# Clustered attention before two expert layers: one-hot tiles turned three at a time, mask rows on 96 partitions, six transfers for two

## What is computed

```python
# attention: B=2, H=8, S=768, D=64, 16 clusters
q_assign = argmax(q_n @ c_n.T)          # cluster of each query, per head
k_assign = argmax(k_n @ c_n.T)          # cluster of each key
mask = q_assign[:, :, :, None] == k_assign[:, :, None, :]
scores = where(mask, scale * q @ k.T, -1e9)
attn = softmax(scores);  out = attn @ v
# experts: N=1536, D=512, E=8, F=1024
idx = argmax(xn @ en.T / tau);  out = gate * (relu(x @ w1[e]) @ w2[e])
# last: d_ff=1536
out = ((x @ w_a) * (x @ w_b)) @ w_out
```

## Time and profile before

| | us |
|---|---|
| median of 3 runs | 868.93 |
| lowest to highest | 867.5 to 874.71 |
| the profiled execution | 872.69 |
| its span, which the profile's times count from | 870.6 |
| PE busy (share of the span) | 823.5 (95%) |
| DVE busy | 424.3 (49%) |
| ACT busy | 288.9 (33%) |
| GpSimd busy | 131.7 (15%) |

### The profile page before, as it was taken

The page is one execution under the profiler, slowest core; times in us unless marked ns, Lnnn a source line. Parts: engine busy times, 40 slices in busy tenths (PEclk is TensorE's granted clock), DMA queues, the critical chain, the costliest instruction groups (busy, mean ns, idle before and its releaser), DMA issues.

```text
span 870.6 us, 13204 instructions
## 1 busy us (share of the span) xinstructions
PE 823.5 (95%) x5441; PEld 748.6 (86%) x5441; DVE 424.3 (49%) x690; ACT 288.9 (33%) x496; POOL 131.7 (15%) x125
## 2 busy tenths in 40 slices
PE   5799999999999999849999999999999999999996
PEld 4589998999989989749999999978888888888885
DVE  5746676776656763258555555544313111131111
ACT  3123323333323343445555555533213111121111
POOL 6001121211111210023333331000001000010001
PEclk9999999999979999859999999999999999999998
DMA  5212222222241101286767677640001000010001
GB/s 135 55 41 60 60 54 70 61 52 60 59 162 41 34 5 56 78 260 188 221 210 216 216 217 216 196 140 7 0 1 49 1 0 1 1 49 0 1 1 48
DMA packets 57471, 72.36 MB, mean 83 GB/s; under 512 B 17696, under 2 KB 40064, under 8 KB 57280
## 3 DMA queue, kind: packets, MB, share of 16 engines
q1 hardware_dynamic: 54624, 63.89, 24.9%
q0 software_dynamic: 2784, 7.58, 2.9%
HBM read 57.24 MB, written 6.30 MB: 73 GB/s over the span
## 4 chain that ended last, share of the span: by engine, by line
PE 90%; DVE 5%; DMA 2%; issue 2%; POOL 1%; ACT 0%; SPq 0%; POOLq 0%; ACTq 0%; DVEq 0%
PE bank L1287 14%; PE bank L1492 8%; PE bank L1494 8%; PE bank L1493 7%; PE pair L1245 5%; PE pair L1451 3%; PE pair L1453 3%; PE pair L1452 3%; PE first_pair L1271 3%; PE bank L1222 3%; PE first_pair L1273 3%; PE bank L1218 2%; PE first_pair L1512 2%; PE first_pair L1510 2%; PE first_pair L1511 2%; PE bank L1512 2%
## 5 line engine op out<-in xcount | busy, mean ns | idle before, releaser
L1287 PE MATMUL bank<-v_sb,prob 128*128 128x66 f32 x1152 | 145.7, 278 | 0.0
L1287 PEld LDWEIGHTS bank<-v_sb,prob 128*128 128x128 f32 x1152 | 144.6, 198 | 0.1
L891 DVE TENSOR_REDUCE neg_max<-pair 128x1 f32<-128x768 f32 x93 | 88.7, 954 | 73.6 <-PE pair L1245 73.5
L1177 DVE TENSOR_TENSOR g_sb<-bank,a_sb 128x512 f32<-128x512 f32 x36 | 24.9, 692 | 187.3 <-PE bank L1494 187.3
L1492 PE MATMUL bank<-x_hi,wt 128*128 128x512 f32 x288 | 112.1, 389 | 1.6 <-DVE x_lo L1158 1.6
L1494 PE MATMUL bank<-x_hi,wt 128*128 128x512 f32 x288 | 112.0, 389 | 0.0
L1493 PE MATMUL bank<-x_lo,wt 128*128 128x512 f32 x288 | 112.0, 389 | 0.0
L651 ACT ACTIVATE prob<-first_pair 128x384 f32<-128x384 f32 x128 | 59.6, 489 | 137.2 <-PE first_pair L1273 136.3
L958 DVE TENSOR_TENSOR wt<-w_raw,wt 128x2048 fp32r<-128x2048 f32 x41 | 93.6, 2287 | 15.7 <-ACT wt L686 15.7
L686 ACT ACTIVATE wt<-w_raw 128x2048 fp32r<-128x2048 f32 x41 | 78.3, 1909 | 1.7 <-DMA w_raw<-in_moe_w_dram 1.1
L1451 PE MATMUL pair<-ht_hi,wt 128*128 128x240 f32 x256 | 71.3, 279 | 0.0
(11 more groups left out here) (229 smaller groups left out, 1625.1 us busy)
## 6 DMA issues: line engine op xcount, KB each, us to landing
w_raw<-in_moe_w_dram SPq DMA_DIRECT2D x32, 1024.0 KB, 9.0
q_raw<-in_q_dram SPq DMA_DIRECT2D x16, 192.0 KB, 2.4
k_raw<-in_k_dram SPq DMA_DIRECT2D x16, 192.0 KB, 2.5
v_sb<-in_v_dram SPq DMA_DIRECT2D x16, 192.0 KB, 3.0
qb<-qa SPq DMA_DIRECT2D x16, 192.0 KB, 2.6
kc<-kd SPq DMA_DIRECT2D x16, 192.0 KB, 2.6
w_raw<-in_moe_w_a_dram SPq DMA_DIRECT2D x3, 1024.0 KB, 7.1
w_raw<-in_moe_w_b_dram SPq DMA_DIRECT2D x3, 1024.0 KB, 8.7
```

Source lines behind the costliest of these rows:

```text
L891: dve.tensor_reduce(neg_max[n % 2][:, t:t + 1], masked_in(n, t)[:, :, 0:HALF], AX.XY, ALU.max, negate=True).then_inc(mx_done, 1)
L1287: last = pe.matmul(o_tiles[:, t, :], prob[s][:, j, t * P:(t + 1) * P], v_in_sb[u][:, j, :], start=(j == 0 and t == 0), stop=(j == NT - 1), ...
```

## The change

Three query tiles and their three key tiles are turned by one transpose: `hot[s][:, 3a:3a+3, :]` is read as 128 x 96, and the result stands on 96 partitions x 128 tokens. Two such transposes fill 96 partitions x 256 columns of the bank, where six filled 32 x 768. Partition 32g + c holds cluster c of the queries of the tiles g and 3 + g, partition 32g + 16 + c that of the keys. `mask_rows` works on 96 x 256 and needs scale and shift on 96 partitions, which the constants now have. `hot_t` becomes 96 x 256. SP sends it in six transfers, three to `qb` and three to `kc`, each of 16 partitions x 2 runs of 128 numbers. `ops_in` now counts 128 a head, and both waits on it are changed to that.

```diff
@@ constants
-    t[0:C, C_MS], t[C:2 * C, C_MS] = 1.0, BIG
-    t[0:C, C_MB], t[C:2 * C, C_MB] = 0.0, -BIG
+    for g in range(3):
+        at = 2 * C * g
+        t[at:at + C, C_MS], t[at + C:at + 2 * C, C_MS] = 1.0, BIG
+        t[at:at + C, C_MB], t[at + C:at + 2 * C, C_MB] = 0.0, -BIG
@@ build
-        hot_t = [sba(f"hot_t{i}", [2 * C, S], F32R) for i in range(2)]
+        hot_t = [sba(f"hot_t{i}", [6 * C, 2 * P], F32R) for i in range(2)]
@@ hot_rows (SP)
-                sp.dma_start(qb[u][D:D + C, :].bitcast(F32), hot_t[s][0:C, :].bitcast(F32)).then_inc(ops_in[u], 16)
-                sp.dma_start(kc[u][D:D + C, :].bitcast(F32), hot_t[s][C:2 * C, :].bitcast(F32)).then_inc(ops_in[u], 16)
+                for g in range(3):
+                    for i, to in enumerate((qb, kc)):
+                        rows = slice((2 * g + i) * C, (2 * g + i + 1) * C)
+                        sp.dma_start(to[u][D:D + C, :].rearrange("c (a g q) -> c a g q", a=2, g=3)[:, :, g, :].bitcast(F32),
+                                     hot_t[s][rows, :].rearrange("c (a q) -> c a q", a=2).bitcast(F32)).then_inc(ops_in[u], 16)
@@ mask_rows (DVE)
-                    dve.wait_ge(ops_in[(n - 2) % 4], 64 * ((n - 2) // 4 + 1))
-                dve.tensor_scalar(hot_t[n % 2][:], at[:, :].bitcast(BF16)[0:2 * C, 0:S], cst[0:2 * C, C_MS:C_MS + 1],
-                                  cst[0:2 * C, C_MB:C_MB + 1], ALU.mult, ALU.add).then_inc(free, 1)
+                    dve.wait_ge(ops_in[(n - 2) % 4], 128 * ((n - 2) // 4 + 1))
+                dve.tensor_scalar(hot_t[n % 2][:], at[:, :].bitcast(BF16)[0:6 * C, 0:2 * P], cst[0:6 * C, C_MS:C_MS + 1],
+                                  cst[0:6 * C, C_MB:C_MB + 1], ALU.mult, ALU.add).then_inc(free, 1)
@@ unit0, unit 5 (PE)
-                    for t in range(NT):
-                        last = pe.transpose(at[:, :].bitcast(BF16)[0:2 * C, t * P:(t + 1) * P], hot[s][:, t, :], ident_bf[:])
+                    for a in range(2):
+                        last = pe.transpose(at[:, :].bitcast(BF16)[0:6 * C, a * P:(a + 1) * P],
+                                            hot[s][:, 3 * a:3 * a + 3, :].rearrange("p t c -> p (t c)"), ident_bf[:])
@@ masked_scores (PE)
-                    pe.wait_ge(ops_in[u], 64 * (n // 4 + 1))
+                    pe.wait_ge(ops_in[u], 128 * (n // 4 + 1))
```

## The result

| | before | after |
|---|---|---|
| median of 4 runs each, us | 871.82 | 908.65 |
| lowest to highest | 867.5 to 876.24 | 905.94 to 924.13 |
| the profiled execution | 872.69 | 911.02 |
| its span | 870.6 | 908.9 |

A forecast was written before the change was run, and what follows sets the result against it. PE was taken to bound the kernel, with each round's masked scores soon waiting for SP's sixth mask transfer. The median 868.9 plus 20.8 us of waits plus 26 for clock falls gave 916 us, range 882 to 952.

The forecast's parts named there:

- The bound and the margin: PE carries the span; at its first masked score the last mask transfer's landing has only 0.36 us to spare.
- mask_rows 0.53 us: DVE's mask_rows step, 96x256 instead of 32x768, would take 0.53 us instead of 1.06.
- An issue every 0.66 us: On SP's queue the six mask transfers would be issued 0.66 us apart, the sixth starting at h + 4.86.
- The landing of 2.0: The sixth mask transfer, 16 KB, would land about 2.0 us after its issue starts; bounds 2.0 and 2.1.
- The transposes' 0.31: On PE, two transposes instead of six would save 0.31 us, bringing PE to the first masked score that much earlier.
- My rival of 864 us: All six transfers land before PE arrives, so shorter transposes gain 13 x 0.31 + 0.8 = 4.8 us; chance 0.05.
- The delay of an undisturbed round: PE's first masked score would start 1.69 us later, at 158.08 instead of 156.39, lengthening the round by that.
- Eleven undisturbed rounds: Eleven of thirteen attention rounds are undisturbed; each would lose 1.69 us, 18.6 us in all.
- The clock: PE's stalls of 2.00 us would lower its clock in half of twelve rounds, 4.4 us each, 26 us.
- The clock holds: Rival: PE's clock never falls and only the waits for transfers are added, 890 us; chance 0.20.
- Falls each time: Rival: PE's clock falls in all twelve rounds, 943 us; chance 0.17, of it 0.04 for a clock staying down.
- The transfers are hidden: Rival: transfers land before PE's first masked score, needing an issue every 0.26 us; not slower, 864 us; chance 0.05.

The follow-up runs named there:

- e4: Kernel before, plus two spare transfers nobody waits for, issued on SP ahead of the two mask transfers from head 3 on: 893.4 us, a single execution.
- e5: Kernel before, plus four spare transfers nobody waits for, issued on SP ahead of the two mask transfers from head 3 on: 941.0 us, a single execution.
- e3: Changed kernel, with the six mask transfers split from head 2 on: three to qb on SP's queue, three to kc on ScalarE's: 867.6 us, 0.9935 times before.
- e8: e3 with four extra 128x32 transposes, results unread, ahead of the two from head 3 on, so PE again turns six: 867.0 us, a single execution.
- e1: Kernel before, with its 32x768 mask rows sent in six transfers; six transposes and the old DVE step stay: 923.5 us, 1.055 times before.
- e6: Kernel before without mask transfers: one-hot tiles padded to 64 columns, VectorE writes query rows and ScalarE key rows straight into the operands: 864.2 us, 0.9927 times before.
- e7: As e6, without mask transfers, but VectorE writes both halves, key rows first: 874.9 us, 1.0063 times before.
- e2: Changed kernel, plus seven extra 96x384 matmuls, results overwritten, on PE ahead of its wait for the transfers: 888.9 us, 1.018 times before.

## Why the prediction held, step by step

**The bound and the margin** held. The landing had 0.36 us to spare, and whatever was put on SP's queue beyond that became PE's wait (e4, e5).

**mask_rows 0.53 us** held: 529 to 540 ns over its 16 instances. The tile `hot_t` of the changed kernel, from its instructions and transfers (count, then min, median and max in ns):

```profile
L926 DVE TENSOR_SCALAR hot_t<-bank,cst x16: 529/530/540, 23.3 to 342.6; 96x256 fp32r<-96x256 bf16 x16
...
L432 SPq DMA_DIRECT2D kc<-hot_t x48: 586/594/1712, 24.7 to 346.4; - x48
...
DMA to landing us min/median/max: 1.8/1.9/3.6
```

**An issue every 0.66 us** was 0.65 on the mean, (4.82 - 1.57) / 5; e4 gives 0.64 by another way. **The landing of 2.0** came out at 1.8 to 1.9: the sixth issue of the quiet round starts at 80.64 and PE at 82.48, 1.84 later where I had 2.05.

**The transposes' 0.31** is one step that failed. The two transposes hold the load queue for 0.10 us (75.93 to 76.03), less than the 0.15 to 0.22 I had bounded them by, and it is free for the next load at h + 0.21 instead of h + 0.57 (151.74 in the earlier trace rows), 0.36 earlier. But it is ready at L1251 at 82.48 - 1.52 = 80.96, h + 5.14, not at my h + 4.91; before, it was h + 5.22. So 0.08 is left of the 0.36. The row of L1293 shows where it went: `times_v` begins at h + 1.16 after a wait of 0.29. The view names no releaser, but in the code it waits for DVE's `token_major`, which reads the bank that `times_v` fills and ends at 76.36 + 0.56 = 76.92. In the kernel before, that end and that start lay close together too, which I didn't look at (timeline of DVE and PEld):

```profile
151.71 0.56 DVE L884 TENSOR_TENSOR x_tok<-bank,weight 128x384 f32<-128x384 f32 x1
...
152.38 1.49 PEld L1287 LDWEIGHTS bank<-v_sb,prob 128*128 128x128 f32 x12
```

152.27 to 152.38 leaves 0.11. My rival of 864 us counted 13 x 0.31 of real gain from this, and its size was wrong for that reason; e3 against e8 measures 0.1 a round with `mask_rows` and transfers out of the way.

**The delay of an undisturbed round**, 1.69, was 1.43 to 1.53 in the five quiet rounds: PE starts at h + 6.66, before at h + 5.22. In the quiet round shown it was 1.44, and the 0.25 that I had too much is 0.21 of landing and 0.04 of issues (h + 4.82 instead of h + 4.86). The failed 0.31 changes PE's stand but not this delay, as the prediction's sum had it: an earlier PE only arrives sooner at the wait.

**"Eleven undisturbed rounds"** is the other step that failed. Before had ten quiet rounds in these twelve; the changed kernel has five. In the other seven PE stands 1.71 to 2.59 us, because one issue or one landing was late. An issue of such a round, SP's timeline:

```profile
140.16 0.59 SPq L432 DMA_DIRECT2D qb<-hot_t  x1
...
140.80 1.66 SPq L432 DMA_DIRECT2D kc<-hot_t  x1
...
142.50 0.59 SPq L432 DMA_DIRECT2D qb<-hot_t  x1
```

The issue of 1.66 is the group's fourth and delays the two behind it by 1.1 us. The DMA view of 140 to 141 us of the changed kernel has a packet of another queue (packets, MB, share of 16 engines):

```profile
q8 instruction: 1, 0.02, 8.4%
```

By its name this is a fetch of the program's own instructions; 8.4% of 16 engines for 1 us is one engine for 1.3 us. From head 2 on the changed kernel has 14 groups of six transfers: in 7 of them such a packet stands beside them, and all 7 have an issue of 1.02 to 1.71 us or a landing of 3.08; in the other 7 there is none, and no issue is over 0.68. e1 shows the same (7 of 7 with one have an issue of 1.00 to 1.59). In e4 seven groups from head 3 on have one: where it stood beside the last transfer, five times, that landed in 3.1 to 3.8 us; where it stood beside the first issues (133.9 and 239.9) one of these took 0.95 and 0.68 and the last landed in 2.1 as always. An eighth, of which the last issue starts at 261.4, landed in 3.2 without a packet, beside bulk loads. In e4's DMA view of 90 to 92 us, the late landing in 3.2 and the packet:

```profile
kc<-hot_t SPq DMA_DIRECT2D x1, 48.0 KB, 3.2
...
q8 instruction: 1, 0.02, 3.1%
```

In the twelve rounds of the kernel before, such a packet stands beside the landing of 3.67 in the earlier trace rows, and one at 227.0 to 228.0 beside an issue that was not late (the 4.79 lay beside bulk loads). With six issues in a row the queue is exposed for 3.8 us a round instead of 1.2, so more fetches should meet it. That they cause the delay is what most of the records suggest; no run here moved the fetches alone, so it isn't shown.

**The clock.** I took half of twelve falls at 4.4 us, 26. Of the twelve stands that I had in mind (head 15's among them) six cost the clock, so the half that I took without a reason was luck; a seventh fall came in the round of 246.54, which answers the one before had already in the earlier trace rows. The size was wrong. The stretch behind a stand, windows of PE alone (length, PE busy, clock, DMA share, GB/s):

```profile
145.00:146.00 1.00, 1.00 (x6) 1.00 0.01 3
146.00:147.00 1.00, 1.00 (x7) 0.62 0.00 0
...
151.00:153.00 2.00, 2.00 (x9) 0.50 0.00 0
153.00:155.00 2.00, 2.00 (x20) 0.98 0.00 0
```

It stood 2.39 us until 144.99, fell (0.50 is 1.2 GHz) near 146.2 and was back near 153, some 6.8 us against the 10 of the earlier trace rows. The round of 137.39 is 24.01 - 18.58 = 5.43 over the quiet one of before, of which the stand is 2.39 and the restart behind it 0.14 (a quiet round's 1.43 less its 1.29): 2.9 is left for the clock. Five falls cost 2.9, one about 2.7, one (224.92) 1.6. My one case was a long one; e3 and e8 have the long one too, in the same place of the kernel (rounds of 25.39 and 25.40). The price goes with the length of the slow stretch, which the rounds' mean clocks give: 0.92 in 21.62 us is 3.5 us at half the clock and cost 1.6; 0.86 in 24.01 is 6.7 and cost 2.9; 0.80 in 25.27 is 10 and cost 4.4. What sets that length stays open; the stand alone does not, for 2.43 us brought the middle one here and 2.27 the long one in e3.

Which stands cost the clock? Over the twelve rounds of all the kernels here but e6 and e7, which don't stand: after a stand of up to 1.11 us it fell in none of 19; after 1.28 to 1.39 in 2 of 6; after 1.61 to 2.81 in 37 of 39 (without e1's unusually long execution in 25 of 27). The quiet rounds of the changed kernel lie in the middle group, the disturbed ones in the last, so what makes a transfer late costs the clock as well as the wait. The Trainium skill (TensorE: Matmul & The Clock Gate, "HAM oscillation") has a kernel in which every tile waits for a DMA and runs slow behind it. By that all twelve would fall; here seven did in the changed kernel, all twelve in e1 and e5, and none in e2, whose stands were filled.

**The sum.** The twelve rounds took 230.68 us before and 265.85 after.

| us | predicted | measured |
|---|---|---|
| more waiting in twelve rounds | 18.6 + 0.5 | 20.6 |
| head 0; head 15, outside the twelve | 1.7; in the eleven | 0.2; 1.8 |
| the clock | 26 | 14.4 |
| not followed | | about 1 |
| sum | 47 | 38.3 (spans) |

The 20.6 is PE's stands of after, 22.46 in all, and 0.14 for the restart of each, 24.1, less the 1.21 and 2.28 of before. The clock is 265.85 - 12 x 18.58 - 24.1 = 18.8, less before's 4.4: six new falls cost 15.9, where I had six at 4.4, and the one that was there before got 1.5 cheaper. Waits of 22.6 against my 20.8 come out right by two errors that cancel: quiet rounds cheaper by 0.2, and more disturbed ones. At head 0 PE stood 2.25 us and started 1.2 later, of which 0.2 was left by the fourth head, as my lower bound of 0 allowed. The round of 244, which I gave neither gain nor loss, got 1.2 shorter (25.27, then 24.06), and not by its wait: its last issue took 1.71 us and PE stood 2.43. Its fall of the clock cost 2.9 instead of 4.4. That stands inside the rows of the table.

**The rivals.** "The clock holds", 890, is what e2 made of it: 889, with the wait filled, and 1.5 us of work is there only for that. "Falls each time", 943, came in no execution of the changed kernel (905.9 to 924.1); the profiled ones of e1 and e5 show it (944.0 and 941.0), the long fall of head 15 included. "The transfers are hidden" fell as its own condition said: an issue would have to come every 0.26 us, and they came every 0.65.

## What to carry to other kernels

Before splitting one transfer into more, lay the issues end to end on the queue that makes them and see when the last starts: here four more meant 2.6 us, seven times the slack, while the work saved on two compute engines was 0.4 and 0.5 us. If the pieces are needed, put them on two queues that stand idle at that moment (e3), or let the engine that reads the data out of PSUM write it to its place (e6), if it has the time just then (e7). And a stand of PE in a loop has two prices, its length and the slower clock behind it; filling it with any work showed which was which (e2).

## What the runs showed of the hardware

- An issue of a small SBUF-to-SBUF transfer holds its queue for 0.59 to 0.66 us and 16 KB land in 1.8 to 1.9, so on one queue the issue of the fourth begins when the first lands.
- Beside a fetch of instructions (16 KB on one DMA engine, 0.9 to 1.6 us) issues in the changed kernel took 1.0 to 1.7 instead of 0.6 us, and landings in e4 up to 3.8 instead of 2.1; a few fetches delayed nothing.
- Stands of 1.3 to 1.4 us already cost the clock in some rounds (2 of 6), those above 1.6 in nearly all (37 of 39), at 2.9 us each as a rule, 4.4 in one place, and 8 to 11 where it fell in head 15.
- DVE and ACT moved 32 partitions x 768 from partitions 0 to 31 or 32 to 63 of PSUM to partitions 64 to 95 of SBUF in 0.95 and 0.89 us, no transfer needed. 96 partitions x 256 took 0.53 where 32 x 768 took 1.06: the time went with the length of the row, not with the partitions.
- The clock's record is not complete at the start: before's first slices read 9, after's 8 and 5, though PE is busy for about the same per matmul from 20 to 46 us in both (19.63 us for 86 and 18.04 for 76). The difference of the mean clocks (0.976 and 0.928) contains that, so I read losses from the lengths of rounds.
- The start varies between the profiled executions: the twelve rounds begin at 75.78 us in before and 75.96 in after, but at 66.26 in e4 and 68.55 in e2, which issue the same as these up to head 3. A single profile's total can be some 9 us off for this reason alone, which is another reason to compare by rounds.
